# The 129th input feature of a fused transform and MLP kernel: spread on TensorE instead of fetched through DRAM

## What is computed

```
X = np.fft.fft(x, axis=1); X = np.fft.fft(X, axis=2); a = X.real      # [2, 3008, 256]
h = a @ w_in;   g = where(h > 0, h, exp(min(h, 0)) - 1);  y = g @ w_out     # 256 -> 2048 -> 256
h = y @ w3;     g = max(h, 0) + alpha * min(h, 0);        out = g @ w4
```

## Time and profile before

| | |
|---|---|
| three runs | 1015.66, 1018.09, 1018.47 us; median 1018.09 |
| profiled execution | 1018.47 us, of it 1016.7 us span from first to last instruction |
| TensorE busy (PE) | 999.1 us, 98% |
| VectorE (DVE), ScalarE (ACT), GpSimd (POOL) | 632.0, 655.6, 89.2 us |
| granted TensorE clock, mean | 0.994 of full |
| TensorE instructions | 4610 matmul records |
| DMA in the first 25 us | 241 GB/s |
| a 256 KB weight piece, DMA issue to landing | 3.1 us |

### The profile page before, as it was taken

One profiled execution on the slowest core, in us unless ns is written; L12 is line 12 of the kernel. 1 busy time (PEld: TensorE's weight loads), 2 busy tenths in 40 slices (PEclk: granted clock), 3 DMA queues, 4 the chain that ended last, 5 costly groups with the idle time before them and its releaser, 6 DMA issues.

```text
span 1016.7 us, 11653 instructions
## 1 busy us (share of the span) xinstructions
PE 999.1 (98%) x4610; PEld 832.2 (82%) x4610; DVE 632.0 (62%) x640; ACT 655.6 (64%) x733; POOL 89.2 (9%) x95
## 2 busy tenths in 40 slices
PE   7979999999999999999999999999999999999997
PEld 6868888888888888878888888888888888888886
DVE  3357887887887887899645445445545545544443
ACT  2247887887787787778766566565555655565554
POOL 3370000000000005860000000000000000000000
PEclk9979999999999999999999999999999999999999
DMA  9420010010010010230020020010002002000101
GB/s 241 132 83 1 1 42 1 1 41 1 1 42 1 1 42 32 63 135 0 1 78 1 1 83 1 1 51 33 0 1 83 1 1 78 1 1 0 42 1 42
DMA packets 8482, 34.59 MB, mean 34 GB/s; under 512 B 1338, under 2 KB 2042, under 8 KB 6508
## 3 DMA queue, kind: packets, MB, share of 16 engines
q1 hardware_dynamic: 5612, 25.03, 7.4%
q0 software_dynamic: 2816, 8.82, 2.9%
HBM read 21.34 MB, written 12.48 MB: 33 GB/s over the span
## 4 chain that ended last, share of the span: by engine, by line
PE 59%; DVE 1%; ACT 0%; issue 0%; DVEq 0%; ACTq 0%
PE ACC L397 11%; PE ACC L402 10%; PE ACC L398 10%; PE PQ L382 8%; PE PQ L381 8%; PE PQ L380 8%; DVE Gl L625 1%; PE PQ L353 0%; PE PQ L354 0%; PE PQ L359 0%; PE PQ L355 0%; PE PQ L358 0%; PE PQ L360 0%; PE PQ L357 0%; DVE H L607 0%; DVE Gl L627 0%
## 5 line engine op out<-in xcount | busy, mean ns | idle before, releaser
L397 PE MATMUL ACC<-Gh,W 128*128 128x512 f32 (+1 forms) x768 | 298.7, 389 | 3.8 <-DVE Gl L625 2.8
L398 PE MATMUL ACC<-Gl,W 128*128 128x512 f32 (+1 forms) x768 | 297.0, 387 | 0.0
L627 DVE TENSOR_TENSOR Gl<-G,Gh 128x1024 fp32r<-128x1024 f32 (+1 forms) x96 | 115.5, 1203 | 214.6 <-ACT Gh L483 214.6
L402 PE MATMUL ACC<-Gh,W 128*128 128x512 f32 (+1 forms) x768 | 234.7, 387 | 0.0
L542 ACT ACTIVATE H<-PQ 128x1024 f32<-128x1024 f32 (+1 forms) x96 | 97.1, 1011 | 131.0 <-PE PQ L382 131.0
L397 PEld LDWEIGHTS ACC<-Gh,W 128*128 128x128 f32 x768 | 144.7, 188 | 38.1 <-issue 4.4
L398 PEld LDWEIGHTS ACC<-Gl,W 128*128 128x128 f32 x768 | 144.8, 188 | 28.0
L402 PEld LDWEIGHTS ACC<-Gh,W 128*128 128x128 f32 x768 | 144.0, 188 | 25.4
L483 ACT ACTIVATE Gh<-G 128x1024 fp32r<-128x1024 f32 (+1 forms) x96 | 100.1, 1042 | 75.2 <-PE ACC L402 71.5
L382 PE MATMUL PQ<-y_hl,W3l 128*128 128x512 f32 (+1 forms) x384 | 147.9, 385 | 0.0
L381 PE MATMUL PQ<-y_hl,W3h 128*128 128x512 f32 (+1 forms) x384 | 147.9, 385 | 0.0
(11 more groups left out here) (70 smaller groups left out, 922.5 us busy)
## 6 DMA issues: line engine op xcount, KB each, us to landing
xr<-in_x SPq DMA_DIRECT2D x16, 384.0 KB, 4.2
raw<-in_w POOLq DMA_DIRECT2D x24, 256.0 KB, 3.1
y_scratch<-y_st SPq DMA_DIRECT2D x5, 1024.0 KB, 3.9
y_in<-y_scratch SPq DMA_DIRECT2D x5, 1024.0 KB, 8.2
out_y<-y_st SPq DMA_DIRECT2D x5, 1024.0 KB, 5.8
wn<-in_wa POOLq DMA_DIRECT2D x4, 256.0 KB, 11.0
wn<-in_wb POOLq DMA_DIRECT2D x4, 256.0 KB, 11.7
out_y<-y_st SPq DMA_DIRECT2D x2, 512.0 KB, 3.3
```

Of the source, the lines that this page charges most:

```text
L397: mm(o, W[:, 0, sl], Gh[:, j, c:c + w], start=f == 0, stop=False)
L398: mm(o, W[:, 0, sl], Gl[:, j, c:c + w], start=False, stop=False)
L402: ins = mm(o, W[:, 1, sl], Gh[:, j, c:c + w], start=False, stop=f == NF - 1)
L627: tt(Gl[:, j, 0:n], G[:, j, 0:n], f32(Gh[:, j, 0:n]), ALU.subtract).then_inc(lo_ready, 1)
```

## The change

The trip through DRAM is gone, and with it `row128` at chunk 10, `e_hl`, the stores, all of `load_e` and the zeroing of `eo(t, 4)`. After the last chunk three matmuls give the row with the 64 points on partitions (`U128`, 64 x 48, copied by ScalarE). Per tile VectorE multiplies it by a 64 x 64 identity, so that eight diagonal blocks stand side by side (`diag`, 64 x 512), and one fp32 matmul with weights of ones (`spread`) gives the row on all 128 partitions in `PQ[:, 1, 0:TW]`. ScalarE copies that to `eo(t, 4)` (`e_hi`), and VectorE writes the low part on partitions 64 to 127 (`e_lo`). The diagonal stands in the place of `eo(t, 4)` that it is to fill. The constant `mcf` grows by the identity and the ones, from 256 to 448 columns.

```diff
-                if c == U_AT:
-                    row128()
                 flip1(c)
...
+            def spread(t):
+                pe.wait_ge(diag_ready, t + 1)
+                if t:
+                    pe.wait_ge(comb_ready, NF * (t - 1) + FLIP_AT)
+                mm(PQ[:, 1, 0:TW], ones, diag[t % 2][:, :], start=True, stop=True).then_inc(e_done, 1)
+
+            pe.wait_ge(cf_in, 16)
+            pe.wait_ge(w1l_ready, 8)
+            pe.wait_ge(t1a_ready, NX)
+            pe.wait_ge(t1b_ready, NX)
+            two = 2 * B * (K2 - 1)
+            o = ACC[:, 0, 0:two // 2]
+            mm(o, m64x[0], T1[N1:PT, 0:two:2, 0], start=True, stop=False)
+            mm(o, m64x[1], T1[N1:PT, 1:two:2, 0], start=False, stop=True)
+            mm(ACC[:, 0, two // 2:two // 2 + B], m64x[0], T1[N1:PT, two:two + B, 0], start=True, stop=True).then_inc(u_done, 1)
             flip2(0)
+            spread(0)
...
             def up1(t, f):
...
                     pe.wait_ge(eol_ready, t + 1)
-                    pe.wait_ge(e_in[t % 2], 48 * (t // 2 + 1))
+                    pe.wait_ge(el_ready, t + 1)
...
+                if t < LAST and f == FLIP_AT + 1:
+                    pe.wait_ge(el_ready, t + 2)
...
                 if f == FLIP_AT and t < LAST:
                     flip2(t + 1)
+                    spread(t + 1)
                     down1(s - 3)
                     up1(t, f)
...
+            def e_hi(t):
+                act.wait_ge(e_done, t + 1)
+                fn(eo(t, 4), PQ[:, 1, 0:TW], ACT.Copy).then_inc(eh_ready, 1)
...
                 if flip_next:
                     eo_hi(t + 1)
+                    e_hi(t + 1)
                     copy_q(s + 1)
...
+            def make_diag(t):
+                u = U128[:, NQ * t:NQ * (t + 1)].unsqueeze(2).to_broadcast([N1, NQ, N1])
+                i = eye.unsqueeze(1).to_broadcast([N1, NQ, N1])
+                tt(diag[t % 2][:, :].rearrange("p (q k) -> p q k", k=N1), u, i, ALU.mult).then_inc(diag_ready, 1)
...
+            def e_lo(t):
+                dve.wait_ge(eh_ready, t + 1)
+                em = eo(t, 4)[PT // 2:PT, :]
+                tt(em, PQ[PT // 2:PT, 1, 0:TW], f32(em), ALU.subtract).then_inc(el_ready, 1)
+
+            dve.wait_ge(cf_in, 16)
+            dve.wait_ge(u_ready, 1)
+            make_diag(0)
             eo_lo(0)
+            e_lo(0)
...
+                if f == FLIP_AT - 3 and t < LAST:
+                    make_diag(t + 1)
                 if f == FLIP_AT - 1 and t < LAST:
                     g_lo(s - 1, -1.0)
                     elu(s)
                     eo_lo(t + 1)
+                    e_lo(t + 1)
```

More of the change, by code:

```diff
@@ L32 @@
 SPLIT_AT = (9, 10, 11, 12)
-U_AT = 10
-U_PARTS = ((B * (K2 - 1), 0), (B, N1))
 FLIP_AT = 8
@@ L40, in program @@
     ALU, ACT = mybir.AluOpType, mybir.ActivationFunctionType
-    e_dram = nc.dram_tensor("e_scratch", [2, B * K2, N1], fp32).ap()
     y_dram = nc.dram_tensor("y_scratch", [NT, PT, YW], fp32).ap()
@@ L68, in program @@
     EO = at("EO", o3, [PT, 2 * EOW], f32r)
+    diag = [at(f"diag{j}", o3 + 4 * (j * EOW + 4 * TW), [N1, TW], fp32) for j in range(2)]
     y_in = at("y_in", o3, [PT, YW], fp32)
@@ L86, in program @@
     o6 = o5 + 16 * KB
-    mcf = at("mcf", o6, [PT, 2 * PT], fp32)
-    e_hl = at("e_hl", o6 + 1024, [C47 // 2, 2, 2, N1], f32r)
+    mcf = at("mcf", o6, [PT, 2 * PT + N1 + PT], fp32)
+    U128 = at("U128", o6 + 1792, [N1, B * K2], fp32)
     warm = at("warm", o6 + 2048, [PT, 1], fp32)
@@ L93, in program @@
     m64x = [mcf[N1:PT, cs * PT:(cs + 1) * PT] for cs in range(2)]
+    eye = mcf[0:N1, 2 * PT:2 * PT + N1]
+    ones = mcf[0:N1, 2 * PT + N1:2 * PT + N1 + PT]
     with ExitStack() as ctx:
@@ L111, in program @@
         f1_done, t1a_ready, t1b_ready = sem("f1_done"), sem("t1a_ready"), sem("t1b_ready")
-        u_done, uh_ready, ul_ready = sem("u_done"), sem("uh_ready"), sem("ul_ready")
-        e_zero, e_stored, e_in = sem("e_zero"), sem("e_stored"), [sem("e_in0"), sem("e_in1")]
+        u_done, u_ready, diag_ready = sem("u_done"), sem("u_ready"), sem("diag_ready")
         f2_done, eoh_ready, eol_ready = sem("f2_done"), sem("eoh_ready"), sem("eol_ready")
+        e_done, eh_ready, el_ready = sem("e_done"), sem("eh_ready"), sem("el_ready")
         q_done, up_done, down_done = sem("q_done"), sem("up_done"), sem("down_done")
@@ L161, in store @@
                     sp.dma_start(d[:, 1, :, 0:m], y_st[:, 1, :, 0:m]).then_inc(y_stored, 16)
[L164 to L178, removed]
             for t in range(NT - 1):
-                if t + 2 < NT:
-                    sp.wait_ge(up_done, NF * (t + 1))
-                    load_e(t + 2)
                 store(y_dram, t, t + 1, TW)
@@ L225, in _ @@
             gp.dma_start(alpha_sb[:, :], alpha).then_inc(alpha_in, 16)
-            for j in range(2):
-                ins = gp.memset(f32(eo(j, 4)), 0.0)
-            ins.then_inc(e_zero, 1)
             chain(gp.memset(f32(W1e[:, :]), 0.0))
@@ L300, in fold_w1 @@
                 mm(o, mcw[:, 1, which, :], wn[:, 1, sl], start=False, stop=True).then_inc(w1_done, 1)
[L303 to L312, removed]
             pe.wait_ge(m47_in, 16)
@@ L457, in _ @@
                     w1_hi(c - 2)
[L458 to L461, removed]
                 t1_copy(c)
+            act.wait_ge(u_done, 1)
+            fn(U128[:, :], ACC[0:N1, 0, 0:B * K2], ACT.Copy).then_inc(u_ready, 1)
             def eo_hi(t):
@@ L509, in _ @@
             eo_hi(0)
+            e_hi(0)
             copy_q(0)
@@ L704, in constants @@
     of_sin = np.block([[-s, -c], [-s, c]])
-    cf = np.concatenate([of_cos, of_sin], 1)
+    cf = np.zeros((PT, 2 * PT + N1 + PT))
+    cf[:, :PT], cf[:, PT:2 * PT] = of_cos, of_sin
+    cf[:N1, 2 * PT:2 * PT + N1] = np.eye(N1)
+    cf[:N1, 2 * PT + N1:] = 1.0
     c, s = cs(np.arange(D), np.arange(PT), D)
```

## The result

The changed kernel took 1023.06 us (median of 5 runs, 1022.25 to 1025.17); the kernel before, in the same rounds, 1017.66 us (1014.96 to 1018.47). The ratio is 1.0065, with a 95% interval of 1.005 to 1.0081, so the change costs 5 to 8 us. (The two medians alone are 5.4 us apart; the record holds 22 runs of the changed kernel, with a median of 1023.27.) In a second set of rounds, with 17 runs of the kernel before, the same program had 1022.74 and a ratio of 1.0054 (1.0039 to 1.007). The forecast was 1022.6, 4.15 us more. The time is as forecast, but the increase was larger than the sum, and the traces show which terms were short.

The account below looks back on a forecast made before the run. TensorE was taken to bound the kernel, its queue full until 434 us. Spread 3.5, start 0.65 and moved matmuls 0.0 summed to 4.15 us on 1018.47, forecasting 1022.6 us, range 1019.0 to 1025.2.

Parts of the forecast that it names:

- What bounds the kernel: Stage 1 until 434 us: TensorE's queue is full, steps take 4.31 us, and added work adds time unless in a gap.
- What is removed: The row's trip through DRAM, with stores, 18 loads and queue wait: hidden, so removing it gives nothing.
- What is moved: The row's three matmuls, 0.66 us, leave their old place and return ahead of flip2(0): net 0.0 (-0.4 to +0.6).
- The spread, the step that was short: One fp32 512-column matmul per tile on TensorE: 0.86 us at each of four flips, 0.07 at the fifth, together 3.5.
- The fifth's gap: At the fifth flip, TensorE's gap of 0.79 us takes in the spread, leaving 0.07 us of its 0.86.
- The two other engines: ScalarE's e_hi and VectorE's e_lo and make_diag inside the loop: covered by idle time and margin, so nothing.
- The start: Ahead of the first up1, e_lo runs behind eo_lo on VectorE without cover: +0.65 us (0.4 to 1.0).
- The sum: Whole kernel: 3.5 + 0.65 + 0.0 = 4.15 us on the profiled execution's 1018.47, giving 1022.6 us, 0.4% more.
- The clock did not stay up by itself: Rival at the start: slow-clock stretches vanish, saving 1.7 and 3.05 us; 1017.9 if neither came, not slower; chance 0.14.
- The cheap spread: Rival at the flips: the spread costs less than an fp32 matmul or finds gaps; one pass gives 1020.0; chance 0.10.
- VectorE was not late at the flips: Rival: make_diag and e_lo make VectorE late, each flip losing up to 1 us more, up to 1027.6; chance 0.14.

Follow-up runs that it names:

- the doubled loads: The kernel before with six 2 KB row loads per tile instead of three, the extra three to partitions with zero weights: 1016.57 us, ratio 1.0001.
- the doubled spread: The changed kernel with the spread matmul issued twice in a row from tile 1 on: 1028.42 us, ratio 1.0113.
- the one-pass spread: The changed kernel with the row kept as high and low parts on 128 rows, summed by one fp32r matmul: 1017.68 us, ratio 1.0012.
- the filled kernel: The kernel before with 10 and 12 idle fp32 matmuls in TensorE's two gaps at the start: 1014.4 us, ratio 0.9976.

## Why the prediction came out as it did

**What bounds the kernel.** Right. Ordinary steps stayed at 4.30 to 4.31 us, and everything added to TensorE's queue up to the last tile appeared in the time one for one.

**What is removed.** Right at nothing, supported by the doubled loads.

**What is moved.** Predicted net 0.0, from 0.66 us taken away. The reading of the earlier trace rows was short: with the held-up chunks on both sides 0.86 us was taken away, and 0.73 came back, so it is -0.13.

**The spread, the step that was short.** The prediction said "0.86 us each" and found little choice, noting that "no row shows that partitions cost anything" and bounding the upper side at 0.95. The matmul itself is 0.87 us, as the doubled spread shows. But a visit costs 1.26, since a matmul with 64 rows among matmuls with 128 pays about 0.36 us for changing over. The one 512-column fp32 matmul of the earlier trace rows has 128 rows and does not show that, but it is not so that no row did: the three 64-row matmuls of the earlier trace rows, the very ones that the change moves, held up their neighbours by 0.2 us. The first of them starts 0.20 us behind the last record of the chunk ahead, and behind them the chunk's second record starts 0.21 us after its first (40.46 to 40.68), where both distances are 0.112 inside a chunk. Four flips and the fifth cost 4 x 1.26 + 0.48 = 5.5 us, not 3.5. The fifth's gap was used up as forecast.

That the Trainium skill (FP8 and Floating Point Precision, TensorE Precision Notes) counts four passes for fp32 agrees with 0.87 against 0.23 us for the one-pass spread; the 131 ns of its page TensorE: Matmul & The Clock Gate (Back-to-back issue gap) is not seen in any stretch, where passes of 512 columns stand 0.215 to 0.227 us apart. (With the 131 ns the prediction's sum would be 4 x 0.52 + 0.65 = 2.7 us, not the "about 2.5" that it names.)

**The two other engines.** Right inside the loop: none of their new operations is waited for, and without the spread the flips return to 10.61. What was not foreseen is VectorE's pause in the last tile, which costs 0.1 to 1.0 us; its cause stays open.

**The start.** Predicted +0.65; 0.80 from flip to first `up1`. `e_lo` runs its full 0.69 us instead of 0.61, and starts behind the end of `eo_lo` (57.80) rather than with an overlap.

**The sum** is then 5.4 (the flips with the steps behind them) + 0.80 - 0.13 = 6.1 us, and 6.2 to 7.1 with the last tile; the two ratios of 1.0065 and 1.0054 make 6.6 and 5.5. That the forecast of 1022.6 lay so near to the measured 1023.06 is in part luck: two errors of opposite sign. The increase of 4.15 was some 2 us short, and it was put on the profiled execution's 1018.47, which stands above the median of before (1017.66, and 1016.51 over more runs) since it had drawn much slow clock (0.994).

**The rivals.** The clock did not stay up by itself: the slow stretches remained in the profiles of the changed kernel, and one of its 22 runs in the first set had a mean clock of 1.000 (1021.25 us), where four of 59 had it before. Work in the two gaps kept it at 1.00 throughout in the filled kernel. That idleness lowers the clock and work restores it, as the Trainium skill has it (TensorE: Matmul & The Clock Gate, What's actually happening), agrees with both. The cheap spread is not what the change has, but it is what the change could have had. VectorE was not late at the flips.

## What to carry to other kernels

Before a fetch is replaced by arithmetic, look for who waits for it: here nobody did, and the bound engine got the new work. A small matmul in a full stream costs its passes and, if it uses another number of rows than its neighbours, a changeover as well; pad it to the same rows and use fp32r halves if the value is split anyway. Where the bound engine has unavoidable gaps at a start, idle matmuls in them can pay, since the work behind the gap then runs at the 2.4 GHz level: here it gave 2.1 us.

## What was not expected of the hardware

A 64-row fp32 matmul between 128-row matmuls costs 1.26 us per visit, 0.90 with 128 rows, at 0.87 us of its own; the three 64-row matmuls of the kernel before show the same on a smaller scale. A VectorE and a GpSimd operation that start within 0.02 us of each other can go either way, 2.21 and 1.28 us or 1.08 and 2.24, from execution to execution of one program; where TensorE waits for VectorE, as in the last tile, this alone is worth about 0.9 us. And the kernel before spreads over 6 us in 35 runs (1013.22 to 1019.61), and most of that goes with the granted clock: over all 59 runs the median is 1014.06 us at a mean clock of 1.000 and 1018.81 at 0.994. The filled one spreads over 2.3 in 12.
